# Attention interleaved with two feed-forward layers on one core: scores with keys on the partitions, maxima and sums over 32x32 blocks on VectorE

## The reference

```python
kv_flat = kv_pool.reshape(B, -1, C) @ w_sr
k = v = kv_flat
s = scale * (q @ k.transpose(0, 2, 1))
s = s - s.max(-1, keepdims=True)
a = np.exp(s)
a /= a.sum(-1, keepdims=True) + 1e-09
x = a @ v
h = x @ w_in                                   # layer 1
g = np.where(h >= 1, h, np.where(h <= -1, 0.0, (h + 1) ** 2 / 4.0))
y1 = g @ w_out
h = y1 @ w_in2                                 # layer 2
g = h * (1.0 / (1.0 + np.exp(-1.702 * h)))
y2 = g @ w_out2
```

## Time and profile before

| | |
|---|---|
| median of three runs | 1369.16 us |
| span of the profiled execution, first to last instruction | 1367.0 us |
| busy: TensorE / VectorE / ScalarE / GpSimd | 97% / 83% / 76% / 13% |
| matmuls and transposes | 6216 |
| 128x1024 subtraction on VectorE | 1217 ns, 384 of them |
| 128x1024 copy on ScalarE | 1054 ns, 384 of them |

### The profile page before, as it was taken

How to read it: one execution, slowest core, us unless ns; L and a number is a source line. 1 busy time by engine, 2 the same in 40 slices (tenths; PEclk the granted TensorE clock), 3 DMA queues, 4 the chain that set the end, 5 groups by cost and what they waited for, 6 DMA issues and landing times.

```text
span 1367.0 us, 18857 instructions
## 1 busy us (share of the span) xinstructions
PE 1331.6 (97%) x6216; PEld 1108.6 (81%) x6216; DVE 1136.5 (83%) x1288; ACT 1033.7 (76%) x1280; POOL 171.4 (13%) x134
## 2 busy tenths in 40 slices
PE   4999999998999999999999999999999999999998
PEld 3888888885888888888888888888888888888886
DVE  6688888889888888888888888888888888888873
ACT  2577777767888787778778787887877787787875
POOL 0666665540000000000000000000000000000000
PEclk9899999999999999999999999999999999999999
DMA  8000000000000000000000000000000000000000
GB/s 324 24 23 23 23 23 23 23 8 1 0 9 8 0 8 8 8 8 0 8 8 8 0 8 8 8 8 0 8 8 8 8 0 8 8 8 0 8 8 16
DMA packets 10143, 23.33 MB, mean 17 GB/s; under 512 B 1040, under 2 KB 1168, under 8 KB 9872
## 3 DMA queue, kind: packets, MB, share of 16 engines
q1 hardware_dynamic: 10128, 23.14, 4.9%
HBM read 16.84 MB, written 6.29 MB: 17 GB/s over the span
## 4 chain that ended last, share of the span: by engine, by line
PE 94%; DVE 2%; SPq 2%; DMA 1%; ACT 1%; issue 0%; POOL 0%; POOLq 0%; ACTq 0%
PE ps_h L284 13%; PE ps_h L286 12%; PE ps_y L284 12%; PE ps_h L285 12%; PE ps_y L286 12%; PE ps_y L285 12%; PE ps_pt L329 5%; PE ps_s L284 3%; PE ps_o L284 2%; PE ps_o L285 2%; PE ps_o L286 2%; PE ps_s L286 2%; PE ps_s L285 2%; SPq L233 1%; DMA w_raw<-in_moe_w_out 1%; DVE g_lo L565 1%
## 5 line engine op out<-in xcount | busy, mean ns | idle before, releaser
L565 DVE TENSOR_TENSOR g_lo<-g,g_hi 128x1024 fp32r<-128x1024 f32 x384 | 467.4, 1217 | 29.2 <-ACT g_hi L432 29.2
L432 ACT ACTIVATE g_hi<-g 128x1024 fp32r<-128x1024 f32 x384 | 389.9, 1054 | 4.3 <-PE ps_y L286 4.1
L482 ACT ACTIVATE g<-ps_h 128x1024 f32<-128x1024 f32 x192 | 197.6, 1029 | 152.3 <-PE ps_h L286 152.3
L284 PE MATMUL ps_y<-g_hi,w_hi 128*128 128x512 f32 x768 | 299.9, 390 | 6.9 <-DVE g_lo L565 4.4
L285 PE MATMUL ps_y<-g_lo,w_hi 128*128 128x512 f32 x768 | 298.9, 389 | 0.0
L286 PE MATMUL ps_y<-g_hi,w_lo 128*128 128x512 f32 x768 | 298.8, 389 | 0.0
L628 DVE SCALAR_TENSOR_TENSOR g<-g 128x1024 f32<-128x1024 f32 x144 | 176.4, 1225 | 91.1 <-ACT g L492 90.9
L492 ACT ACTIVATE g<-ps_h 128x1024 f32<-128x1024 f32 x192 | 197.7, 1030 | 59.9 <-PE ps_h L286 52.4
L641 DVE TENSOR_TENSOR g<-ps_h,g 128x1024 f32<-128x1024 f32 x192 | 233.8, 1218 | 0.0
L284 PEld LDWEIGHTS ps_y<-g_hi,w_hi 128*128 128x128 f32 x768 | 144.3, 188 | 40.9 <-DVE g_lo L565 7.3
L286 PEld LDWEIGHTS ps_y<-g_hi,w_lo 128*128 128x128 f32 x768 | 144.1, 188 | 30.2
(11 more groups left out here) (57 smaller groups left out, 1587.1 us busy)
## 6 DMA issues: line engine op xcount, KB each, us to landing
kv_sb<-in_kv_t SPq DMA_DIRECT2D x12, 512.0 KB, 8.2
q_sb<-in_q_t SPq DMA_DIRECT2D x24, 256.0 KB, 2.6
out_t<-y_sb SPq DMA_DIRECT2D x24, 256.0 KB, 2.0
w_raw<-in_moe_w_in SPq DMA_DIRECT2D x2, 1024.0 KB, 17.4
wsr_sb<-in_w_sr SPq DMA_DIRECT2D x1, 64.0 KB, 1.8
w_raw<-in_moe_w_out SPq DMA_DIRECT2D x2, 0.5 KB, 13.8
```

The costliest lines, as they stand in the source:

```text
L284: nc.tensor.matmul(dst, l_hi, r_hi, start=start, stop=False)
L432: return nc.scalar.activation(dst, src, ACT.Copy, scale=scale)
L482: nc.scalar.activation(g2[:, uu % 2, :], ps_h2[:, :], ACT.Gelu_apprx_sigmoid).then_inc(g2_done, 1)
L565: return nc.vector.tensor_tensor(dst, src, upper.bitcast(F32), ALU.subtract)
```

## The change

The two phases become one loop of 28 iterations. Iteration `it` begins with a block of chunks on TensorE (6 chunks of scores of tile `it`, 6 chunks of values of tile `it-2`), followed by eight feed-forward steps, in which layer 1 works 18 steps and layer 2 29 steps behind. `layer_out` of layer 2 now runs one step after its `layer_in` instead of two.

The scores have the keys on the partitions, 128 keys by 512 queries a chunk. DVE copies each chunk out of PSUM to `s_sb`. The maximum over the keys, now across partitions, is a `tensor_reduce` with `apply_transpose` over 32x32 blocks, then six small DVE operations that bring the four groups of 32 partitions together and turn the result. SP writes the 512 maxima to DRAM and reads them back broadcast to 128 partitions (`key_max`). DVE subtracts them (`shift`, three operations of 1024 a tile), ACT takes the exponential without bias. The sums go the same way (`add_keys`, `invert`, `inv_sum`) and multiply the output of the values instead of the probabilities (`normalise`). TensorE has no transposes, and nothing is held for a whole phase: `x_t` is gone.

In a feed-forward step, ACT makes `g2_hi` by a second gelu from PSUM, and squares in all units; DVE writes `g1_hi` and `g1` by two operations with h in PSUM; POOL makes `g1_lo`, `g2_lo` and `q_lo` instead of DVE. The three slots of PSUM for h1 and h2 are a ring that the scores and values share. Three tiles are handled by separate code at the start (`RAMP`), in which ACT copies the scores; there ACT and POOL split the weights.

The core of the diff, the new parts:

```diff
+        ps_ring = ps(ctx, "ps_ring", [P, 3, UW])
+        ps_y1 = ps(ctx, "ps_y1", [P, T])
+        ps_y2 = ps(ctx, "ps_y2", [P, T])
+        def ps_s(c):
+            return ps_ring[:, 0, (c % 2) * T:(c % 2 + 1) * T]
+        ps_o = ps_ring[:, 1, 0:T]
+        def ps_h2(k):
+            return ps_ring[:, (2 + 2 * k) % 3, :]
+        def ps_h1(k):
+            return ps_ring[:, (3 + 2 * k) % 3, :]
...
+        LAG1, LAG2 = 2, 1
+        FIRST1, FIRST2 = 18, 29
...
+            def spread_max(t):
+                sp.wait_ge(max_turned_done, t + 1)
+                sp.dma_start(max_row, max_turned[0:QB, :]).then_inc(max_stored, 16)
...
+                at_least(sp, shifted, t * PAIRS)
+                sp.dma_start(key_max[:, :], max_row.rearrange("j i -> (j i)").partition_broadcast(P)).then_inc(max_spread, 16)
...
+            def step(it, k):
+                exists, tt, uu, n = unit(it, k, FIRST2)
+                if exists:
+                    slot = uu % 2
+                    pool.wait_ge(g2_hi_done, n + 1)
+                    at_least(pool, g2_used, n - 1)
+                    nc.gpsimd.tensor_tensor(g2_lo[:, slot, :], g2[:, slot, :], g2_hi[:, slot, :].bitcast(F32),
+                                            ALU.subtract).then_inc(g2_lo_done, 1)
+                exists, tt, uu, n = unit(it, k, FIRST1)
+                if exists:
+                    slot = uu % 2
+                    pool.wait_ge(g1_done, n + 1)
+                    at_least(pool, g1_used, n - 1)
+                    nc.gpsimd.tensor_tensor(g1_lo[:, slot, :], g1[:, slot, :], g1_hi[:, slot, :].bitcast(F32),
+                                            ALU.subtract).then_inc(g1_lo_done, 1)
+            def iteration(it, half):
+                for k in range(U):
+                    step(it, k)
+                    if k == 3 and is_tile(it + 1):
+                        q_lower(it + 1, 1 - half)
...
+            def block_of_chunks(it):
+                score_chunk(it, 0)
+                score_chunk(it, 1)
+                value_chunk(it, 0)
+                value_chunk(it, 1)
+                value_chunk(it, 2)
+                score_chunk(it, 2)
+                value_chunk(it, 3)
+                score_chunk(it, 3)
+                value_chunk(it, 4)
+                score_chunk(it, 4)
+                value_chunk(it, 5)
+                score_chunk(it, 5)
...
+                    act.wait_ge(h2_ready, n + 1)
+                    at_least(act, g2_lo_done, n - 1)
+                    nc.scalar.activation(g2[:, slot, :], ps_h2(k), ACT.Gelu_apprx_sigmoid).then_inc(g2_done, 1)
+                    at_least(act, g2_used, n - 1)
+                    nc.scalar.activation(g2_hi[:, slot, :], ps_h2(k),
+                                         ACT.Gelu_apprx_sigmoid).then_inc(g2_hi_done, 1)
+                exists, tt, uu, n = unit(it, k, FIRST1)
+                if exists:
+                    act.wait_ge(h1_ready, n + 1)
+                    at_least(act, g1_lo_done, n - 1)
+                    g = g1[:, uu % 2, :]
+                    nc.scalar.activation(g, ps_h1(k), ACT.Relu, bias=0.5, scale=0.5).then_inc(relu_done, 1)
+                if k == 3 and is_tile(it - 3):
+                    act.wait_ge(g1_used, (it - 3) * U + U)
+                    at_least(act, h2_ready, (it - 4) * U)
+                    copy(y1_hi[:, 1 - half, :], ps_y1[:, :]).then_inc(y1_hi_done, 1)
...
+            def iteration(it, half):
+                if is_tile(it - 1):
+                    for p in range(PAIRS):
+                        exponential(it - 1, 1 - half, p)
+                    for p in range(PAIRS):
+                        probs_upper(it - 1, 1 - half, p)
+                if is_tile(it - 2):
+                    x_upper(it - 2, half)
+                for k in range(U):
+                    step(it, half, k)
...
+                nc.vector.tensor_copy(s_sb[:, half, c, :], ps_s(c)).then_inc(s_evac, 1)
+            def fold(dst, g):
...
+                return nc.vector.tensor_copy(dst[0:SQ, g, :], dst[g * SQ:(g + 1) * SQ, 0, :])
...
+                nc.vector.tensor_reduce(part_max[:, chunks, :],
+                                        s_sb[:, slot, chunks, :].rearrange("p c (j i) -> p c j i", i=SQ), axis=AX.X,
+                                        op=ALU.max, apply_transpose=True).then_inc(part_max_done, 1)
...
+            def shift(t, slot, p):
+                dve.wait_ge(max_spread, t * 16 + 16)
+                pair = s_sb[:, slot, 2 * p:2 * p + 2, :]
+                nc.vector.tensor_tensor(pair, pair, key_max[:, :].unsqueeze(1).to_broadcast([P, 2, T]),
+                                        ALU.subtract).then_inc(shifted, 1)
+            def add_keys(t, slot, p):
+                chunks = slice(2 * p, 2 * p + 2)
+                dve.wait_ge(exp_done, t * PAIRS + (p + 1))
+                nc.vector.tensor_reduce(part_sum[:, chunks, :],
+                                        s_sb[:, slot, chunks, :].rearrange("p c (j i) -> p c j i", i=SQ), axis=AX.X,
+                                        op=ALU.add, apply_transpose=True).then_inc(part_sum_done, 1)
...
+            def unit_upper(it, k):
+                exists, tt, uu, n = unit(it, k, FIRST1)
+                if exists:
+                    dve.wait_ge(square_done, n + 1)
+                    at_least(dve, g1_used, n - 1)
+                    nc.vector.scalar_tensor_tensor(out=g1_hi[:, uu % 2, :], in0=g1[:, uu % 2, :], scalar=1.0,
+                                                   in1=ps_h1(k), op0=ALU.min, op1=ALU.max).then_inc(g1_hi_done, 1)
+            def unit_full(it, k):
+                exists, tt, uu, n = unit(it, k, FIRST1)
+                if exists:
+                    g = g1[:, uu % 2, :]
+                    nc.vector.scalar_tensor_tensor(out=g, in0=g, scalar=1.0, in1=ps_h1(k), op0=ALU.min,
+                                                   op1=ALU.max).then_inc(g1_done, 1)
+            def step(it, half, k):
+                if k == 3 and is_tile(it - 3):
+                    dve.wait_ge(y1_hi_done, it - 2)
+                    lower(y1_lo[:, 1 - half, :], ps_y1[:, :], y1_hi[:, 1 - half, :]).then_inc(y1_lo_done, 1)
+                unit_upper(it, k)
+                if k < U - 1:
+                    unit_full(it, k)
+                if is_tile(it):
+                    if k == 0:
+                        maximum(it, half, 0)
+                    if k == 1:
+                        maximum(it, half, 1)
+                        maximum(it, half, 2)
+                    if k == 2:
+                        fold_maximum(it)
+                    if k == 4:
+                        shift(it, half, 0)
+                    if k == 6:
+                        shift(it, half, 1)
+                    if k == 7:
+                        shift(it, half, 2)
+                if is_tile(it - 1):
+                    if k == 3:
+                        add_keys(it - 1, 1 - half, 0)
+                    if k == 5:
+                        add_keys(it - 1, 1 - half, 1)
+                        add_keys(it - 1, 1 - half, 2)
+                    if k == 6:
+                        invert(it - 1)
+            def iteration(it, half):
+                evacuate(it, half, 0)
+                evacuate(it, half, 1)
+                unit_full(it - 1, U - 1)
+                for c in range(2, KC):
+                    evacuate(it, half, c)
+                if is_tile(it - 2):
+                    normalise(it - 2)
+                if is_tile(it - 1):
+                    for p in range(PAIRS):
+                        probs_lower(it - 1, 1 - half, p)
+                if is_tile(it - 2):
+                    x_lower(it - 2, half)
+                for k in range(U):
+                    step(it, half, k)

```

More of the change, by code:

```diff
@@ L97, in encoder_kernel @@
[L97 to L108, removed]
+        with ExitStack() as raw:
+            kv_sb = sb(raw, "kv_sb", [C, NK, WIN])
@@ L429, in _ @@
+            for c in range(KC):
+                value_chunk(2, c)
+            for c in range(KC):
+                score_chunk(2, c)
+            for k in range(U):
+                step(2, 0, k)
+            iterations(pe, iteration)
         @block.scalar
@@ L449, in _ @@
+            def iteration(it, half):
[6 more added lines that the diff above has]
+                    x_upper(it - 2, half)
+                for k in range(U):
+                    step(it, half, k)
+            q_upper(0, 0)
             k_upper(0)
@@ new lines, in _ @@
+            for p in range(PAIRS):
+                probs_upper(0, 0, p)
+            w_upper(1)
+            w_upper(2)
+            evacuate(2, 0)
+            step(2, 0, 2)
+            exponential(1, 1, 0)
+            exponential(1, 1, 1)
+            step(2, 0, 3)
+            exponential(1, 1, 2)
+            probs_upper(1, 1, 0)
+            step(2, 0, 4)
+            probs_upper(1, 1, 1)
+            probs_upper(1, 1, 2)
+            step(2, 0, 5)
+            step(2, 0, 6)
```

(47 more changed lines are left out.)

741 lines of the change are left out of this document (349 added, 392 removed).

## The result

Three timed rounds and the profiled execution of the changed kernel give a median of 1553.76 us (1552.35 to 1554.34), against 1369.00 for the kernel before on the same chip: ratio 1.1342, interval 1.1328 to 1.1356. The forecast was 1350, its range 1322 to 1408. It is a miss by 204 us and in sign.

What follows compares the result with a forecast made beforehand. TensorE, busy 97%, was taken as the bound: 1238 us of matmuls, 76.5 of gaps at the start and 13 of tail make 1327.5; 20 of stalls and 2.2 from span to median give 1350, range 1322 to 1408.

Steps and rivals of the forecast that it cites:

- fourteen small ones by the 0.14 of a one-element row: In DVE's sum for an iteration: fourteen small operations at 0.14 us each, plus waits, 2.8 of 40 us.
- if small copies take over 1 us: One of the signs named beforehand that would show the forecast wrong: small copies longer than 1 us.
- s: TensorE's stall in each of the 20 iterations between start and tail: taken as 1.0 us, 20 us in all; break-even 2.0.
- DVE becomes the bound: Rival: the transposing reduction takes 2.4 us, or small operations wait for POOL in steps 2 and 6; 1430 us; chance 0.05 each.
- at once: End of an iteration: the last shift goes in without waiting for POOL, and TensorE stalls 0.2 us.
- with the wait: End of an iteration: the last shift waits 2.3 us for POOL, stall 2.8; every time, 1386 us; its rival's chance 0.33.
- half chance: Last shift of an iteration: even odds of waiting for POOL or not would give a stall of 1.5 us; 1.0 was taken.
- Start and tail: Start: iteration 4 begins near 143 us, with 76.5 of gaps; tail: last ten steps at 3.6 us each, 13 in all.
- the wait of two SBUF inputs: On DVE: an operation with two SBUF inputs waits for POOL's to end; three shifts, three pt_lo and x_lo have two.
- forecast iteration of 52.6: Expected length in us of one of the 20 middle iterations, where TensorE's work alone is 51.6.
- The drain of 1380 ns: ACT's table switches: a skill's extra cost beside the 1.28 us load, left out of the forecast; would add 20 us.

Runs made afterwards that it cites:

- m1: A kernel of its own, computing nothing of the reference: POOL subtractions run beside seven forms of DVE operation; all but the reduction wait, about 2.34 us beside the small forms.
- e1: The changed kernel with its six small fold copies a tile made reductions over an axis of length one: 1380.22 us, 1.0073 of before.
- e3: On top of e1, the added 1e-9 becomes a fifth summand of the sums' last reduction, with a longer fold_sum tile: 1387.75 us, 1.0132 of before.
- e5: On top of e4, a tile's last shift moved behind the first two copies of the next tile's scores: 1358.62 us, 0.9924 of before.
- e7: On top of e1 alone, the last shift moved behind the first two copies of the next scores: 1361.01 us, 0.9937 of before.
- e4: On top of e3, two of the sums and the second shift moved to earlier steps: 1385.98 us, 1.0117 of before.
- e8: On top of e5, the last eleven g2_lo of layer 2 made on DVE instead of POOL: 1353.04 us, 0.9877 of before.

## Why the prediction failed, step by step

- **The step that failed** is "fourteen small ones by the 0.14 of a one-element row", in DVE's sum. Six of the fourteen are SBUF copies of 16 elements and measured 1.5 us, 9.0 an iteration. The sign "if small copies take over 1 us" came true. The row was the wrong neighbour: an added scalar of one element a partition shows no wait beside POOL, and one of 16 does (161 ns to 1.99 us in the kernel after, 2.26 in m1). I used the same row a second time to give this rival 0.05, though it was named with its place and its 2.4 us each.
- **The rival's own price was too low, and its name was wrong.** It had s = 5; it is 61.4 - 51.6 = 9.8. I called it "DVE becomes the bound", but DVE is busy 325 of 400 us: it is late in two places. I counted the delay on DVE, not what it sets off: 6.0 of idle TensorE and 3.1 slow by the windows above (together 9.1 of the 9.8), at most 2.4 of it by the clock. By the windows of before the clock is low only near the start; the gaps of 3.5 us and some of those of 2.1 bring the lower level back, those of 1.5 in e1 do not.
- **The error as a sum.** Iterations 20 x (61.4 - 52.6) = 176. The rest of the span is 1552.5 - 20 x 61.4 = 324.5 against 1327.5 + 20 - 20 x 52.6 = 295.5, 29 more. Between median and span are 1.3, not 2.2. Together 204.
- **The last shift.** I chose s = 1.0 between "at once" and "with the wait" and said that it hung on 0.1 us. e1 is the walk with the wait: 53.5 an iteration against my 54.4, and 1380 against 1386. There was no half chance: the last shift waits in every iteration of e1 and of e3 (medians 1.81 and 2.83 us).
- **Start and tail.** Iteration 4 starts at 144 in e5 (forecast 143); in the changed kernel `max_turned` of tile 4 comes 22 later than in e5. The steps of the tail take 3.75 against 3.6. The fixed part is 308.7 in e5, 13 over my 295.5, and it lies at the end: behind iteration 23, from 1192.1 on, e5 takes 165.0 us where the forecast has 1347.5 - 1195 = 152.5. The tail was priced too low; which of its waits make the 12 us is not worked out.
- **What held.** TensorE's work: 5496 matmuls on the page with those of the projection (5472 forecast), no transposes, and in e5 a pace of 0.230 without a wait. POOL's subtraction (2.4 forecast, 2.41 measured in the median), the transposing reduction (1.22, 1.226), the round trip of the maxima (1.3 + 3.4 = 4.7 us, forecast 5), the wait of two SBUF inputs read from the earlier trace rows. With both waits away the forecast iteration of 52.6 is 52.4, and 1350 stands against 1358.6 (e5) and 1361.0 (e7). That the iteration agrees is in part luck: the forecast has 1.0 us of stall in it, e5 has none and a slower matmul instead.
- **The table loads** cost their row alone: in e1 `x_hi` ends at 746.53, a load starts at 746.55 and takes 1.28, and the gelu starts at 747.85. The drain of 1380 ns that the Trainium skill adds (ScalarE: Activation LUTs, "What ACT_TABLE_LOAD costs") is seen neither ahead of it nor behind it, so the 20 us that I worked out by it did not come.

Not shown: the share of the lower clock by an experiment of its own, since it went together with the gaps and 2.4 us is a bound from one trace; and what makes the feed-forward matmuls slower from e3 on.

## What to carry to other kernels

When work is moved to GpSimd, every operation of VectorE beside it needs its kind checked, and a small size is no excuse: a copy of 16 elements a partition waited up to 2.3 us, nearly all of GpSimd's 2.4. Price a small operation by a row of the same kind, shape and neighbour; where there is none, put its full wait into the forecast and not into a rival with 0.05. And before a wait is taken away, look which operation comes next: put it where the other engine is idle, or the wait only moves. When an edit that removes a wait makes the kernel slower, look at the waits first: if they fell, as in e3, count the matmuls of a stretch without gaps.

## What the runs showed of the hardware

- A reduction over an axis of length one copies 32x16 elements in 0.157 us beside a busy GpSimd, where a copy takes 2.26.
- The wait goes both ways: GpSimd's 128x1024 subtraction takes 3.33 to 3.39 us instead of 2.41 where it meets a 1.22 us shift.
- A destination with a stride does not free a copy of the wait (2.26 us).
- At the full granted clock and without gaps, feed-forward matmuls of 512 columns took 0.2306 us each in e3, e4, e5 and e8, and 0.2267 to 0.2272 in the other kernels (175 against 178 in 40 us, e3 and e1); the cause is open.
